# Stores of split weights issued earlier in the attention head, and another timetable for the high halves that ScalarE makes in the third and fourth tile

## What is computed

```python
for c in range(768 // 32):                      # chunks of 32 queries
    k_ctx = k[:, :, max(0, 32*c - 16) : min(768, 32*c + 40)]    # v_ctx likewise
    k_full, v_full = concat(mem_k, k_ctx), concat(mem_v, v_ctx)
    a = softmax(q_c @ k_full.T / sqrt(64))
    out[:, :, 32*c : 32*c + 32] = a @ v_full
x = out.transpose(0, 2, 1, 3).reshape(3072, 512)
h = x @ w_in0;  x = elu(h) @ w_out0             # 3072x512 @ 512x2048, then 2048x512
h = x @ w_in1;  x = (s * relu(h)**2 + b) @ w_out1
```

## Time and profile before

| | |
|---|---|
| median of three runs | 1204.31 us |
| profiled execution, its time | 1202.13 us |
| its span, first to last instruction | 1200.4 us |
| mean granted TensorE clock | 0.975 of full speed |
| TensorE matmul busy | 92% |
| VectorE, ScalarE, GpSimd busy | 71%, 64%, 35% |
| moved by DMA | 302.81 MB, 252 GB/s |

### The profile page before, as it was taken

How to read it: one execution, slowest core, us unless ns; L and a number is a source line. 1 busy time by engine, 2 the same in 40 slices (tenths; PEclk the granted TensorE clock), 3 DMA queues, 4 the chain that set the end, 5 groups by cost and what they waited for, 6 DMA issues and landing times. The chain is left out here.

```text
span 1200.4 us, 18155 instructions
## 1 busy us (share of the span) xinstructions
PE 1109.2 (92%) x5787; PEld 880.0 (73%) x5787; DVE 847.8 (71%) x1234; ACT 767.4 (64%) x1799; POOL 425.1 (35%) x458
## 2 busy tenths in 40 slices
PE   8977498988999999989999899899999999999998
PEld 4755376766777777768788678687887887888876
DVE  4875079746976874897874996948957549667385
ACT  4966276767566775856756667656666466666464
POOL 4487867746222231224454525654101000200000
PEclk8997799999999999999999999999999999999999
DMA  9996799999889898769999869997678666776664
GB/s 198 251 258 191 210 360 291 310 342 292 246 240 268 223 285 248 232 214 325 356 293 294 277 192 371 312 351 255 179 224 267 193 193 189 204 228 186 192 190 158
DMA packets 204055, 302.81 MB, mean 252 GB/s; under 512 B 112824, under 2 KB 121016, under 8 KB 203960
## 3 DMA queue, kind: packets, MB, share of 16 engines
q1 hardware_dynamic: 203960, 301.65, 83.0%
HBM read 226.10 MB, written 75.50 MB: 251 GB/s over the span
## 5 line engine op out<-in xcount | busy, mean ns | idle before, releaser
L985 PE MATMUL ps<-xc_hi,w_ring 128*128 128x512 f32 x1344 | 434.8, 396 | 18.8 <-ACT s L1134 13.2
L1000 PE MATMUL ps<-g_hi,w_ring 128*128 128x512 f32 x1344 | 424.3, 397 | 23.6 <-issue 15.1
L1000 PEld LDWEIGHTS ps<-g_hi,w_ring 128*128 128x128 f32 x1344 | 250.0, 190 | 86.7 <-issue 25.1
L985 PEld LDWEIGHTS ps<-xc_hi,w_ring 128*128 128x128 f32 x1344 | 254.1, 189 | 75.5 <-issue 15.1
L1000 PE MATMUL ps<-g_lo,w_ring 128*128 128x512 f32 x672 | 263.9, 393 | 0.0
L985 PE MATMUL ps<-xc_lo,w_ring 128*128 128x512 f32 x672 | 263.3, 392 | 0.0
L772 POOL TENSOR_TENSOR w_new<-w_raw,w_new 128x256 fp32r<-128x256 f32 x182 | 165.5, 912 | 210.4 <-ACT w_new L1217 207.0
L1440 DVE TENSOR_TENSOR g_lo<-X,g_hi 128x512 fp32r<-128x512 f32 x240 | 188.5, 791 | 51.7 <-ACT g_hi L1203 51.3
L1203 ACT ACTIVATE g_hi<-X 128x512 fp32r<-128x512 f32 x240 | 149.4, 628 | 77.2 <-PE ps L1000 74.5
L1357 DVE TENSOR_TENSOR X<-s,ps 128x512 f32<-128x512 f32 x144 | 96.0, 681 | 92.0 <-ACT s L1140 67.0
L1000 PEld LDWEIGHTS ps<-g_lo,w_ring 128*128 128x128 f32 x672 | 127.5, 190 | 27.3
(11 more groups left out here) (116 smaller groups left out, 1388.1 us busy)
## 6 DMA issues: line engine op xcount, KB each, us to landing
w_ring<-w_scratch SPq DMA_DIRECT2D x336, 512.0 KB, 4.5
w_scratch<-w_new SPq DMA_DIRECT2D x182, 256.0 KB, 5.0
w_scratch<-att SPq DMA_DIRECT2D x42, 256.0 KB, 4.9
w_raw<-in_moe_w_in SPq DMA_DIRECT2D x16, 512.0 KB, 5.7
w_raw<-in_moe_w_out SPq DMA_DIRECT2D x16, 512.0 KB, 5.5
x_scratch<-y SPq DMA_DIRECT2D x12, 512.0 KB, 6.4
att<-x_scratch SPq DMA_DIRECT2D x12, 512.0 KB, 6.6
out<-elu SPq DMA_DIRECT2D x24, 256.0 KB, 4.3
```

Source lines behind the costliest of these rows:

```text
L985: last = nc.tensor.matmul(bank_of(st.pi, st.i), w[:, a, cols], x[:, st.pi, kk, :], start=(st.pi in (P1, P5, P4) and kk == 0 and n == 0), s ...
L1000: last = nc.tensor.matmul(bank_of(st.pi, d), w[:, a, cols], x[:, k % RING, :], start=(st.pi in (P1, P5) + (P4,) * (1 - st.gr) and st.i == ...
```

## The change

The head's stores are issued earlier: two after the loads of each of the units 4 to 8, then up to number `2 * it + 12` in iteration `it` but not over 28; two more after `save_x0(HEAD - 4)` and two after `save_x0(HEAD - 3)`. Stores 32 to 41 follow two for each `d`, and are no longer asked for all in d = 4. ScalarE's first high half (`pp` 42) moves from step 4 to step 12 of the first tile, and one follows every 0.95 step in place of every 1.1. In tiles 2 and 3 the 42 high halves lie in steps 7 to 20 and 36 to 82, one every 1.5 steps; before they lay in steps 2 to 92 of tile 2 (every 2.2) and 8 to 73 of tile 3 (every 1.6).

```diff
-HEAD_SAVES = 28
+HEAD_SAVES = 32
@@ def hi_slot(pp):
     if pp < PRODUCTS:
-        return 4 + (pp - HEAD_PREP) * 11 // 10 + (3 if pp >= PREP_AT[PAIR + 1, P1] else 0)
+        return 12 + (pp - HEAD_PREP) * 19 // 20 + (3 if pp >= PREP_AT[PAIR + 1, P1] else 0)
     if pp < WIDE_END:
         return PER_TILE + 4 + (pp - PRODUCTS) * 3
-    if pp < WIDE_END + 42:
-        return 2 * PER_TILE + 2 + (pp - WIDE_END) * 11 // 5
-    return 3 * PER_TILE + 8 + (pp - WIDE_END - 42) * 8 // 5
+    t, j = divmod(pp - WIDE_END, 42)
+    return (2 + t) * PER_TILE + (7 + j * 3 // 2 if j < 10 else 36 + (j - 10) * 3 // 2)
@@ def saves_due(d):
-    return max(min(HEAD_PREP, HEAD_SAVES + 2 * (d - W_RING + 1)), HEAD_PREP + sum(at // 2 + 4 <= d for at in HI_SLOT.values()))
+    early = HEAD_SAVES + 2 * (d - W_RING + 1)
+    return early if early < HEAD_PREP else HEAD_PREP + sum(at // 2 + 4 <= d for at in HI_SLOT.values())
@@ block.sync, the loads of units 0 to 8
                 if n in (0, 2):
                     load_raw(n // 2)
+                while saves < 2 * (n - 3):
+                    save_weights(saves)
+                    saves += 1
@@ the head's loop
-                while saves < min(HEAD_SAVES, 2 * it + 2):
+                while saves < min(HEAD_SAVES - 4, 2 * it + 12):
                     save_weights(saves)
                     saves += 1
                 if 12 <= it < 12 + W_RING:
                     load_weights(it - 12)
             save_x0(HEAD - 4)
+            while saves < HEAD_SAVES - 2:
+                save_weights(saves)
+                saves += 1
             sp.dma_start(sb_scalars[:, 0:1], s_in.partition_broadcast(128)).then_inc(scalars_in, 16)
             sp.dma_start(sb_scalars[:, 1:2], b_in.partition_broadcast(128)).then_inc(scalars_in, 16)
             save_x0(HEAD - 3)
+            while saves < HEAD_SAVES:
+                save_weights(saves)
+                saves += 1
```

## The result

The changed kernel takes 1176.32 us (median of four, 1174.72 to 1179.09), the kernel before, on the same chip, 1205.88: a ratio of 0.9755, 95% interval 0.9724 to 0.9787. The forecast was 1173, range 1160 to 1188. The profiled execution took 1176.55 us (span 1174.8), 25.6 less than the one before; the forecast's sum was 30.9. It lies at its kernel's median, while the one of before lay 2 to 4 under its own, so the medians differ by more (29.6) than the traces that are compared here.

The account below looks back on a forecast made before the run. TensorE is busy 92% of the span; only its idle and half-clock time can be won, mostly two holes where engines wait for stores. -15.7 - 17 + 4 - 2.2 = -30.9 us gives 1173 us, range 1160 to 1188.

Parts of the forecast that it names:

- First hole: Head, TensorE's 14.0 us wait at 82 us: earlier stores leave about 1 us of it; step 0 15.7 us earlier.
- choice of 0 for ten stores ahead of the loads: Head: ten stores ahead of unit loads delay unit 16's keys by 0 us; 1.6 at the slower DMA rate.
- Second hole: Steps 0 to 13, TensorE's 13.2 us wait at 125.7: 27.5 us in place of 48.3, 20.8 won.
- The wait that moves to step 12: First tile: `cut_w` waits in step 12 for stores 40 and 41, ScalarE 7 to 9 us; loss 3.8.
- Rest of the first tile: First tile with denser high halves: GpSimd late, DMA full; loss of 4 us, bounds 0 and +8.
- Tiles 2 and 3: New timetable of high halves around the down phases: 2.2 us won in sum, bounds -8 and +5.
- Step 28: Fourteen steps from step 28: fewer VectorE operations beside GpSimd; tile 2 -2.8 us, tile 3 -3.8.
- Step 84: Four GpSimd sums in steps 83 to 88 slow VectorE by 4.3 us: tile 2 -0.6, tile 3 +4.
- (a): Second hole stays in part: ScalarE's 9 us in step 12 reach TensorE, first tile gives back 12; 1185 us, chance 0.18.
- (b): Head falls into step with the stores: 5 us in seven rounds, keys late by 1.6; 1180 us, chance 0.1.
- (c): Slower: store landings above 9.6 us cost 35 us over seven rounds of the head; 1208 us, chance 0.06.
- (d): No change: both holes reappear at the next wait because DMA bounds the first tile; chance 0.06.

Follow-up runs that it names:

- e4: e1 without the early stores of the head: later stores and later `cut_w` alone; 1194.27 us, ratio 0.9904 to the kernel before.
- e2: The kernel before with only the new timetable of high halves in tiles 2 and 3; 1201.65 us, ratio 0.9960.
- e1: The changed kernel with the high halves of tiles 2 and 3 where they were before; 1178.49 us, ratio 0.9769 to the kernel before.
- e3: The kernel before with only the early stores of the head; 1193.49 us, ratio 0.9888.
- e5: The changed kernel, with GpSimd's first four sums of activations for tiles 3 and 4 waiting until step 94; 1171.43 us, ratio 0.9721 to the kernel before.
- e9: The changed kernel, with those four sums made one by one behind the weight sets of steps 36 to 72; 1168.53 us, ratio 0.9681 to the kernel before.
- e10: The changed kernel with one high half every step of the first tile, not every 0.95, still from step 12; 1178.36 us, ratio 0.9769.
- e11: e9 with e10's slots: sums spread and one high half a step in the first tile; 1166.49 us, ratio 0.9673 to the kernel before.
- e6: The changed kernel with ScalarE's split that waits for GpSimd's first sum in head iteration 15, not 14; 1177.63 us, ratio 0.9786.
- e7: The changed kernel with the edits of e5 and e6 together; 1171.90 us, ratio 0.9725 to the kernel before.
- e8: The changed kernel with ScalarE's first high half in step 15, not 12, and one every 0.9 step; 1177.63 us, ratio 0.9780.

## Why the prediction was right, and where its terms were off

The mechanism was the one forecast, and the sum was 5.3 us too large on the traces (30.9 against 25.6).

**First hole: -12.0, forecast -15.7.** The hole begins at 81.75, at 82.0 before, so the choice of 0 for ten stores ahead of the loads came out, but by luck. From 36 to 82 us TensorE worked 43.28 us of 46 with 494 matmuls, before 45.26 with 522, and came to the same place: it had been ahead at 36, where the granted clock from 20 to 36 us was 1.00 and before 0.89. What it was ahead it lost, 1.9 us of it in three waits for the loads of keys, which the kernel before doesn't have. Over all traces the hole begins at 80.8, 81.8 and 82.0 with the late stores (e4, e2, before) and at 80.5 to 83.7 with the early ones (the change, e1, e3, e5, e9, e10, e11; e6 and e7 split otherwise there), and once, in e8, at 87.2: 1.5 us later in the mean. So this term is nearer to 1.5 us than to 0, by traces that differ by more than that. Two other parts were off in the two traces themselves. TensorE waits 2.44 us in place of 1: 1.4. From there to step 0 it takes 13.1 us where the even pace makes 10.6: 2.5, of which the stretch from 84 to 91.9 at a granted clock of 0.57, nearly 1.2 GHz throughout, is the visible part. The prediction took the half clock for a result of a 14 us hole that would go with it. e6 shows that taking the wait away does not bring all of this: its clock is 1.00, and other waits take its place.

**Second hole: steps 0 to 13 -20.6, forecast -20.8.** As forecast: 27.8 us in place of 27.5, the loads of unit 17 in time, no long wait. e3 and e4 show that this gain is that of the later stores and the later `cut_w`, by itself.

**The wait that moves to step 12: +5.9, forecast +3.8.** The first high half runs at 128.9, forecast 120 to 124. GpSimd was later: its sums began at 81.7 as forecast, but product 41 ended at 127.1 in place of 120. The list of waits has 5.3 us of this: five times it waited for the landing of a store, the last time 2.4, and the prediction had it run from product to product at 13.3 us a set. ScalarE stood for 6.1 us and TensorE's cover held in part: the wait at the place named, for ScalarE's copy into PSUM, is 2.17 (TensorE was there at 131.2, forecast 124.8), the other 3.4 us of idle time lie in small waits around it (30.20 less 24.63 is 5.57 in all, 0.72 before). By e8, which takes 4.6 us of the wait away, these 14 steps have 4.2 us to give.

**Rest of the first tile: +3.3, forecast +4.** The tile gives back 4.9 up to step 56 and takes 1.6 again later. Neither of the two other spacings tried, e8 and e10, is better.

**Tile 1: +1.3, forecast nothing.** The high halves there are as before. The tile takes 197.8 us here, 196.5 before and 195.1 in e1, whose tile 1 is the same. It goes with the number of short stretches at the lower clock: three here, two before and none in e1, so 0.7 to 0.9 us each. This is scatter between executions.

**Tiles 2 and 3: -3.5, forecast -2.2.** Step 28 was worth -4.1 and -5.2 in place of -2.8 and -3.8: both stretches reach 19.1, the pace of matmuls alone, where I had left a rest. The prediction's +1 for steps 7 to 20 is +1.6 (steps 14 to 27 of tile 2, 20.8 us at a DMA share of 1.03 and 391 GB/s, with waits for ring loads). Step 84 was the term that was mis-sized: in tile 2 +1.6 in place of -0.6, in tile 3 +5.1 in place of +4. Its two parts were off in opposite directions. Four sums at 1.07 made 4.3 in the forecast, from one operation of the earlier trace rows; the rows show 3.2 (0.50, 0.52, 1.07 and 1.07), since an operation that meets a sum near its end loses less, and TensorE's idle time grew by 3.1. What was left out is the lower clock that follows the idle time, 2.4 us. In tile 2, where the four sums stood before too, idle time grew by 0.8 and busy time by as much. e5 takes the sums away and leaves the dense high halves, and step 84 falls to 20.9 us: the sums set this place, and the high halves that were moved away from it had not. Small gains elsewhere, 1.1 us in steps 70 to 83 of tile 3 the largest, bring the two tiles to -3.5.

The stretch of 391 GB/s, like those of the earlier trace rows, is above the 358 GB/s that the Trainium skill gives for a core in "DMA: Bandwidth & Descriptors", section "Where 436 GB/s comes from". By it tile 2 should have lost 2 more; the trace shows 1.6 in all.

Of the rivals, (a), that the second hole stays in part, has its trace here, 2.1 us of the 12 it would have given; (b), a head late by 5 us before the hole, is not in the change's trace, where the hole begins on time; e8's trace, the same code up to there, has a head of that size, 5.2 us late, with 4.3 us of waits for keys. (c) and (d) are out.

## What to carry to other kernels

A queue that one engine issues in a hand-written order is worth reading before any engine's busy share: both long holes were waits for stores that stood behind loads or in a bunch. A wait that a high-priority edit takes away comes back at the next thing that is late, so follow the chain to that point and price it, here 5.9 of 32.5 us. Before other work is thinned out at the narrow place of a phase, look at what really lies in it: the four sums of GpSimd in one piece cost more there than all the products that were moved, and one at a time elsewhere they cost almost nothing.

## What the runs showed of the hardware that was not expected

- *The clock after a short wait.* After 4.57 us of idle time TensorE ran at 1.2 GHz for about 4.8 us, after 2.44 us in the head for about 8 us (granted 0.57). The same wait of the head is 2.4 us in e5, 2.0 in e11 and 2.3 to 3.3 in e1, e3, e9 and e10, and each time a stretch at a granted clock of 0.50 to 0.51 begins within 4 us of its end. In e8 a wait of 1.63 us that ended at 92.4 is followed by a granted clock of 0.50 until 100. In e6, with waits of 1.0 and 1.2 us, it stayed at 1.00. But the wait of 2.17 us at 133.4 in the change, and that of 1.96 us at 96.1 in e6, have 1.00 behind them. So a wait of 1.6 us or more can be followed by the lower clock and need not be; what else decides it was not tried.
- *A head that differs between executions.* With the same code up to there, step 0 begins at 97.2 us in the change, 97.5 in e5, 96.6 in e1, 99.4 in e9 and 103.0 in e8. The waits for keys differ with it: 1.9 us in the change, 4.3 in e8. The order of transfers with full DMA engines is a possible reason, and was not tested. It is as large as most single terms of the forecast, so one trace can't confirm such a term to a microsecond.
- *VectorE beside GpSimd.* The same operation takes 0.68 us alone, up to 1.22 beside GpSimd's products and 1.75 beside its sums of 128x512. The Trainium skill ("SBUF — State Buffer", section "Who interferes with whom") calls the port between them an exclusive lock for the whole instruction. The rows agree with it. GpSimd's last sum runs from 810.68 to 812.28; VectorE's operation begins at 811.07 and ends at 812.82, 0.54 later. The one of 806.58 ends at 807.76, 0.55 behind the first sum's end at 807.21. In the whole trace of the change 202 VectorE operations of 128x512 with both operands in SBUF begin while a GpSimd instruction runs; the middle 80% of them end 0.54 to 0.55 us behind its end. The 70 such operations with one operand in PSUM take 0.67 to 0.69 us. So the price of one meeting is what is left of GpSimd's instruction, less 0.13 us or so, and four sums with hardly a gap between them can cost several operations in a row.
